# Tuned two-MLP kernel on one Trainium2 core: pairs of token tiles with a lag of three pairs

## What is computed

```python
kv = np.einsum('bhsd,bhse->bhde', k_s, v)          # k_s: softmax over the positions
x  = np.einsum('bhsd,bhde->bhse', q_s, kv)         # q_s: softmax over the columns

h = x @ w_in;  g = np.maximum(h, 0) + alpha * np.minimum(h, 0)
x = g @ w_out

h = x @ w_in2
e = np.exp(h - max(h));  sm = e / (sum(e) + 1e-9)
solu = h * sm
ln = (solu - mean(solu)) / sqrt(var(solu) + 1e-6) * g_ln
out = ln @ w_out2
```

## Time and profile before

| | |
|---|---|
| median of 3 runs | 1238.48 us (1237.42 to 1242.6) |
| profiled execution | 1237.77 us, its span 1236.0 us |
| PE busy in the span | 1196.8 us (97%) |
| DVE, ACT, POOL busy | 909.0 (74%), 537.1 (43%), 310.0 us (25%) |
| ninth chunk's down product | ends at 832.6 us |
| periods of stage 3 | from 832.6 us, the last one begins at 1179.94 us |

### The profile page before, as it was taken

One profiled execution on the slowest core, in us unless ns is written; L12 is line 12 of the kernel. 1 busy time (PEld: TensorE's weight loads), 2 busy tenths in 40 slices (PEclk: granted clock), 3 DMA queues, 4 the chain that ended last, 5 costly groups with the idle time before them and its releaser, 6 DMA issues.

```text
span 1236.0 us, 16164 instructions
## 1 busy us (share of the span) xinstructions
PE 1196.8 (97%) x6013; PEld 988.3 (80%) x6013; DVE 909.0 (74%) x1165; ACT 537.1 (43%) x744; POOL 310.0 (25%) x233
## 2 busy tenths in 40 slices
PE   7999999999999999999999999997889999999997
PEld 6778887878788888888888888985667888888886
DVE  7869678686773577869777686754789888888872
ACT  4443434434353334444434444333454554545441
POOL 5632413224141000000000000124543545353400
PEclk9999999999999999999999999998899999999999
DMA  9797787878865654270642704693355454544333
GB/s 229 226 283 261 238 258 232 249 249 261 268 191 181 236 198 172 74 237 35 196 145 85 238 17 161 207 293 105 125 166 171 150 156 155 152 159 151 135 128 111
DMA packets 211918, 225.07 MB, mean 182 GB/s; under 512 B 63208, under 2 KB 148224, under 8 KB 211712
## 3 DMA queue, kind: packets, MB, share of 16 engines
q1 hardware_dynamic: 206064, 212.50, 54.7%
q0 software_dynamic: 5728, 11.53, 3.3%
q10 hardware_dynamic: 48, 0.01, 0.0%
HBM read 128.51 MB, written 95.48 MB: 181 GB/s over the span
## 4 chain that ended last, share of the span: by engine, by line
PE 77%; DVE 8%; DMA 4%; issue 4%; POOL 2%; SPq 2%; ACT 2%; POOLq 0%; DVEq 0%; ACTq 0%
PE ps_y L1840 8%; PE ps_y L1842 7%; PE ps_y L1841 7%; PE ps_y L1926 5%; PE ps_y L1928 5%; PE ps_y L1930 5%; PE ps_y L1984 5%; PE ps_y L1985 5%; PE ps_y L1986 5%; PE ps_m L1926 3%; PE ps_m L1928 3%; PE ps_m L1930 2%; PE ps_m L1965 2%; PE ps_m L1969 2%; PE ps_m L1967 2%
## 5 line engine op out<-in xcount | busy, mean ns | idle before, releaser
L1840 PE MATMUL ps_y<-X,W 128*128 128x512 f32 x576 | 226.7, 394 | 0.0
L1842 PE MATMUL ps_y<-X,W 128*128 128x512 f32 x576 | 224.4, 390 | 0.0
L1841 PE MATMUL ps_y<-X,W 128*128 128x512 f32 x576 | 224.3, 389 | 0.0
L1364 DVE SCALAR_TENSOR_TENSOR gst<-gst,nslope,ps_y 128x512 f32<-128x512 f32 x144 | 104.4, 732 | 111.0 <-ACT gst L967 110.6
L967 ACT ACTIVATE gst<-ps_y 128x512 f32<-128x512 f32 x144 | 85.7, 596 | 224.8 <-PE ps_y L1842 166.1
L836 POOL TENSOR_TENSOR x2r<-x2r 128x256 f32<-128x256 f32 x18 | 25.1, 1394 | 410.0 <-DMA x2r<-x_scratch 410.0
L1984 PE MATMUL ps_y<-WO,zh 128*128 128x512 f32 x288 | 115.3, 400 | 11.9 <-DVE zl L1665 11.9
L1840 PEld LDWEIGHTS ps_y<-X,W 128*128 128x128 f32 x576 | 108.1, 188 | 23.1
L1842 PEld LDWEIGHTS ps_y<-X,W 128*128 128x128 f32 x576 | 108.1, 188 | 22.8
L1841 PEld LDWEIGHTS ps_y<-X,W 128*128 128x128 f32 x576 | 108.1, 188 | 22.0
L1926 PE MATMUL ps_y<-rh,WOc 128*128 128x512 f32 (+1 forms) x320 | 118.6, 371 | 3.0 <-DVE rl L1526 2.9
(11 more groups left out here) (189 smaller groups left out, 2519.5 us busy)
## 6 DMA issues: line engine op xcount, KB each, us to landing
g_scratch<-gst SPq DMA_DIRECT2D x144, 256.0 KB, 3.5
RX<-g_scratch SPq DMA_DIRECT2D x36, 512.0 KB, 3.6
z_scratch<-zb SPq DMA_DIRECT2D x36, 512.0 KB, 2.7
zt<-z_scratch SPq DMA_DIRECT2D x144, 128.0 KB, 2.9
ws_scratch<-whl SPq DMA_DIRECT2D x22, 512.0 KB, 4.5
RY<-g_scratch SPq DMA_DIRECT2D x18, 512.0 KB, 4.0
RZ<-g_scratch SPq DMA_DIRECT2D x18, 512.0 KB, 4.6
x2r<-x_scratch SPq DMA_DIRECT2D x18, 512.0 KB, 5.0
```

Of the source, the lines that this page charges most:

```text
L1364: nc.vector.scalar_tensor_tensor(gst[:, n % 3, :], gst[:, n % 3, :], nslope[:, f:f + 1], ps_y[:, f % 4, :], ALU.mult, ALU.add).then_inc(g_ ...
L1840: nc.tensor.matmul(o, W1[:, f, 0, a, :], x[:, 0, a, :], start=(a == 0), stop=False)
L1841: nc.tensor.matmul(o, W1[:, f, 0, a, :], x[:, 1, a, :], start=False, stop=False)
L1842: mm = nc.tensor.matmul(o, W1[:, f, 1, a, :], x[:, 0, a, :], start=False, stop=(a == KT - 1))
```

## The change

- TensorE's period n becomes: blocks 0 to 3 of pair n, m2 of (n-3, 0), blocks 4 to 6, m2 of (n-3, 1). Three pairs are behind at the end.
- h has three sets of buffers (hs[n % 3]; h20, h21 are new), so the waits on solu_ok go back three pairs.
- The first five periods of ACT, DVE, POOL and SP stand in another order, and the loops are one pair further behind: DVE's is now zt_low(n-3,0), form_early(n), norm(n-2,0), norm(n-2,1), zt_low(n-3,1), form_12(n), form_21(n), max(n-1,0), max(n-1,1), solu(n-1,0), solu(n-1,1).
- x2r1 and x2lb1 change places in memory. load_x2(1) is issued once the low part of unit (3,1) of the ninth chunk is made; x2_sums(1) stands ahead of load_wo2 on POOL; x2_high(0) comes behind product 2, x2_high(1) behind unit (6,0).
- The ninth chunk's units use three slots. In it DVE does v and c22 behind the low part of unit (4,0), and b_turn of product 4 behind the low parts of product 5.

```diff
-                self.slot = 1 + s % 2 if self.single else r % 3
-                if self.single:
-                    self.before = r - 2 if s >= 2 else r - 3
-                else:
-                    self.before = r - 3
+                self.slot = r % 3
+                self.before = r - 3
...
+                if u == PAIRS:
+                    sp.wait_ge(bl_ok, number(PAIRS, 3, 1) + 1)
+                    load_x2(1)
                 store_x2(u, 3, p1, c22_ok, 2 * (u + 1), y22_st)
...
+            for n in range(5, PERIODS + 4):      # SP
+                if n - 4 < PERIODS:
+                    store_out(n - 4, 1)
+                if n - 2 < PERIODS:
+                    store_z(n - 2, 0)
+                    load_z(n - 2, 0)
+                if n - 3 < PERIODS:
+                    store_out(n - 3, 0)
+                if n - 2 < PERIODS:
+                    store_z(n - 2, 1)
+                    load_z(n - 2, 1)
                 if n + 3 < PERIODS:
                     load_x2(n + 3)
...
             x2_low(0)
+            x2_sums(1)
             load_wo2(0)
             load_wo2(1)
-            x2_sums(1)
             x2_low(1)
             x2_sums(2)
             x2_low(2)
+            x2_sums(3)
             power(0, 0)
-            x2_sums(3)
             x2_low(3)
+            x2_sums(4)
             power(0, 1)
-            x2_sums(4)
+            x2_low(4)
+            x2_sums(5)
             power(1, 0)
-            x2_low(4)
             power(1, 1)
-            x2_sums(5)
+            x2_low(5)
+            x2_sums(6)
             power(2, 0)
             power(2, 1)
-            x2_low(5)
-            x2_sums(6)
-            power(3, 0)
-            power(3, 1)
-            for n in range(5, PERIODS):
-                power(n - 1, 0)
-                power(n - 1, 1)
+            for n in range(5, PERIODS + 2):
+                power(n - 2, 0)
+                power(n - 2, 1)
                 if n + 1 < PERIODS:
                     x2_low(n + 1)
                 if n + 2 < PERIODS:
                     x2_sums(n + 2)
...
+            for n in range(5, PERIODS + 4):      # ACT
+                if n - 2 < PERIODS:
+                    square_tile(n - 2, 1)
+                if n < PERIODS:
+                    first_copy(n)
+                if n - 4 < PERIODS:
+                    out_copy(n - 4, 1)
+                if n - 3 < PERIODS:
+                    zt_high(n - 3, 1)
                 if n + 1 < PERIODS:
                     x2_high(n + 1)
+                if n - 3 < PERIODS:
+                    out_copy(n - 3, 0)
+                if n < PERIODS:
+                    h11_copy(n)
+                if n - 2 < PERIODS:
+                    zt_high(n - 2, 0)
+                if n - 1 < PERIODS:
+                    exp_tile(n - 1, 0)
+                    exp_tile(n - 1, 1)
+                    square_tile(n - 1, 0)
...
+                if t.u == LAST_U and t.k == 4:
+                    if t.j == 0:
+                        post("v", t.u)
+                        post("c22", t.u)
+                    continue
+                if t.u == LAST_U and t.k == 5:
+                    b_turn(UNITS[number(t.u, 4, t.j)])
...
             tile_solu(0, 0)                      # DVE, the first periods
             form_early(1)
-            tile_solu(0, 1)
+            norm_tile(0, 0)
             form_12(1)
             form_21(1)
-            norm_tile(0, 0)
+            form_early(2)
+            tile_solu(0, 1)
+            zt_low(0, 0)
...
+            for n in range(5, PERIODS + 3):
+                zt_low(n - 3, 0)
+                if n < PERIODS:
+                    form_early(n)
+                if n - 2 < PERIODS:
+                    norm_tile(n - 2, 0)
+                    norm_tile(n - 2, 1)
+                zt_low(n - 3, 1)
+                if n < PERIODS:
+                    form_12(n)
+                    form_21(n)
+                if n - 1 < PERIODS:
+                    tile_max(n - 1, 0)
+                    tile_max(n - 1, 1)
+                    tile_solu(n - 1, 0)
+                    tile_solu(n - 1, 1)
...
                 if n >= 3:
-                    m2_product(n - 3, 1)
+                    m2_product(n - 3, 0)
                 for k in range(4, PARTS):
                     m1_product(n, k)
-                if n >= 2:
-                    m2_product(n - 2, 0)
-            m2_product(PERIODS - 3, 1)
-            for n in range(PERIODS - 2, PERIODS):
+                if n >= 3:
+                    m2_product(n - 3, 1)
+            for n in range(PERIODS - 3, PERIODS):
                 for t in range(2):
                     m2_product(n, t)
```

More of the change, by code:

```diff
@@ L112, in linear_attention_two_mlps @@
         h00, h01 = place(RAW_AT + 4096, ("h00", [P, F2], F32), ("h01", [P, F2], F32))
-        zl, p1c, h11t = place(RAW_AT + 6144, ("zl", [P, 2, F2], F32R), ("p1c", [P, TOK], F32), ("h11t", [P, F2], F32))
+        zl, p1c, h11t, h20, h21 = place(RAW_AT + 6144, ("zl", [P, 2, F2], F32R), ("p1c", [P, TOK], F32), ("h11t", [P, F2], F32),
+                                        ("h20", [P, F2], F32), ("h21", [P, F2], F32))
         ps_y = ctx.enter_context(nc.psum_tensor("ps_y", [P, 4, TOK], F32))
@@ L1113, in _ @@
                         c11_copy(t.u)
-                    if t.u == LAST_U and t.k == 4:
+                    if t.u == LAST_U and t.k == 2:
                         x2_high(0)
+                if t.u == LAST_U and t.k == 6 and t.j == 0:
+                    x2_high(1)
             def first_copy(n):
@@ L1168, in _ @@
             exp_tile(0, 0)
+            x2_high(2)
             first_copy(1)
             exp_tile(0, 1)
-            x2_high(2)
             square_tile(0, 0)
             h11_copy(1)
-            square_tile(0, 1)
+            x2_high(3)
             first_copy(2)
-            x2_high(3)
-            exp_tile(1, 0)
             h11_copy(2)
             zt_high(0, 0)
+            square_tile(0, 1)
+            first_copy(3)
+            x2_high(4)
+            exp_tile(1, 0)
             exp_tile(1, 1)
+            zt_high(0, 1)
@@ L1181, in _ @@
             square_tile(1, 0)
-            zt_high(0, 1)
             square_tile(1, 1)
-            first_copy(3)
+            h11_copy(3)
             out_copy(0, 0)
-            x2_high(4)
+            x2_high(5)
             exp_tile(2, 0)
+            first_copy(4)
+            zt_high(1, 0)
             exp_tile(2, 1)
-            zt_high(1, 0)
             out_copy(0, 1)
             square_tile(2, 0)
-            h11_copy(3)
+            zt_high(1, 1)
             square_tile(2, 1)
-            zt_high(1, 1)
+            out_copy(1, 0)
@@ L1195, in _ @@
+            h11_copy(4)
             exp_tile(3, 0)
-            first_copy(4)
-            out_copy(1, 0)
             exp_tile(3, 1)
-            x2_high(5)
+            zt_high(2, 0)
             square_tile(3, 0)
[L1201 to L1213, removed]
+            for n in range(5, PERIODS + 4):
[7 more added lines that the diff above has]
+                    zt_high(n - 3, 1)
@@ L1679, in _ @@
             form_early(1)
-            tile_solu(0, 1)
+            norm_tile(0, 0)
             form_12(1)
             form_21(1)
-            norm_tile(0, 0)
+            form_early(2)
+            tile_solu(0, 1)
+            zt_low(0, 0)
+            form_12(2)
+            form_21(2)
+            norm_tile(0, 1)
+            form_early(3)
             tile_max(1, 0)
-            form_early(2)
-            norm_tile(0, 1)
-            zt_low(0, 0)
             tile_max(1, 1)
             tile_solu(1, 0)
-            form_12(2)
@@ L1691, in _ @@
-            form_21(2)
             tile_solu(1, 1)
+            zt_low(0, 1)
+            norm_tile(1, 0)
+            form_12(3)
+            form_21(3)
+            norm_tile(1, 1)
             tile_max(2, 0)
             tile_max(2, 1)
-            zt_low(0, 1)
-            norm_tile(1, 0)
-            form_early(3)
-            norm_tile(1, 1)
             tile_solu(2, 0)
             zt_low(1, 0)
+            form_early(4)
             tile_solu(2, 1)
-            form_12(3)
-            form_21(3)
@@ L1734, in _ @@
-            n = PERIODS - 1
-            norm_tile(n, 0)
-            norm_tile(n, 1)
-            for t in range(2):
-                zt_low(n - 1, t)
-            for t in range(2):
-                zt_low(n, t)
+            tile_max(3, 0)
+            tile_max(3, 1)
+            tile_solu(3, 0)
+            tile_solu(3, 1)
+            for n in range(5, PERIODS + 3):
[14 more added lines that the diff above has]
+                    tile_solu(n - 1, 1)
```

119 lines of the change are left out of this document (25 added, 94 removed).

## The result

The changed kernel takes **1276.11 us**, the median of 4 runs (1275.45 to 1277.93), beside 1237.95 for the kernel before (1235.40 to 1242.60): ratio 1.031 (95% interval 1.027 to 1.034). It is slower. 1280 in a range of 1240 to 1292 was forecast. The profiled execution took 1275.84 us with a span of 1274.0, 38.0 more than the 1236.0 of before.

What follows compares the result with a forecast made beforehand. TensorE was taken as full through 950 to 1190 us, so only stalls at start and end could be won. 1236.0 - 11.4 (start) + 46.0 (middle) + 7.1 (end) = 1277.7 us of span, stated as 1280, range 1240 to 1292.

Steps and rivals of the forecast that it cites:

- Ninth chunk, +0.7: At unit (4,1), DVE's rl waits for POOL's x2_low(0); TensorE idles 3.6 us in place of 2.9: +0.7 us.
- Start, -25.5 and what is late next: Second pair sooner removes the old start's 25.5 us of stalls; new ones come; start in sum -11.4 us.
- Both new stalls: Start: m2(1,0) waits for zl in period 4, +4.9 and 2.4 clock; m1(2,1) waits for form_12, +4.0 and 1.7.
- Middle, +46.0: Periods 5 to 16: x2_low holds tensor_scalar, zl is late, TensorE idles 2.7 us each, 32.4, plus 13.6 of slow clock.
- the clock's share: Middle: two of three stalls also draw the slow clock, 12 x 1.1 = 13.6 us.
- The bound that only adds 0.41 to tensor_scalar: Middle: tensor_scalar only grows by 0.41, zl is 0.75 us late per period, 9 us in all.
- the second rival: Middle: only the growth of 0.41, zl 0.75 us late per period, total 1242; chance 0.09.
- the first rival: Middle: POOL loses the race, tensor_scalar starts first, zl 1.5 us late, 18 in all, total 1251; chance 0.11.
- x2_low late enough: Middle: rival in which x2_low begins behind zt_low and holds nobody, TensorE never waits, total 1228; chance 0.15.
- End, +7.1: Last products: zl(15,0) and m2(16,0) come late, 11.1 us with slow clock against 4.0 before: +7.1 us.
- m2(16, 0)'s 4.2: End: m2(16,0) waits behind norm(16) twice, maxima and solu of 17: 4.2 us idle.
- The sum, 1279.5: Whole kernel: span 1277.7 us from all terms, 1279.5 for the profiled execution, stated as 1280.

Runs made afterwards that it cites:

- Experiment 6: Changed kernel with load_x2(1), x2_sums(1) and x2_high(1) put back where they stood before the change: 1287.63 us, ratio 1.041.
- experiment 8: experiment 3 plus ACT's exp ahead of zt_high, power(0,0) ahead of x2_sums(3), and x2_low(5) waiting for norm(1,1): 1230.96 us, ratio 0.995.
- experiment 1: Changed kernel, but POOL's x2_low(n+1) waits until DVE's second norm has its e: 1255.65 us, ratio 1.015.
- Experiment 9: experiment 8 with the last period and the end written out in a new order on DVE, ACT and SP: 1220.44 us, ratio 0.987.
- experiment 5: Changed kernel with x2_low as two operations of seven rows each, nothing between them: 1252.49 us, ratio 1.012.
- 10 to 12: x2_low(0), x2_low(1) in four pieces: on Experiment 9 1224.20 us, on the changed kernel 1276.22, on Experiment 9 with waits between pieces 1223.38.
- experiment 11: Changed kernel with x2_low(0) and x2_low(1) in four pieces, nothing between them: 1276.22 us, ratio 1.031.
- experiments 2: Changed kernel with DVE's zt_low(n-3,1) ahead of the two norms: 1255.42 us, ratio 1.014.
- experiment 3: Changed kernel with the edits of experiment 1 and experiments 2 together: 1246.83 us, ratio 1.008.

## Why the prediction was right

By position: unit (4, 0) of the ninth chunk and the first blocks of pairs 5 and 17 begin, in the changed kernel, at

```profile
813.69 0.28 PE L1898 MATMUL ps_m<-rh,WOc 128*128 128x256 f32 x1
...
916.52 0.39 PE L1937 MATMUL ps_m<-W2c,x2hb 128*128 128x512 f32 x1
...
1203.74 0.39 PE L1937 MATMUL ps_m<-W2c,x2hb 128*128 128x512 f32 x1
```

and in the kernel before (pair 17 at 1179.94) at

```profile
810.71 0.28 PE L1926 MATMUL ps_m<-rh,WOc 128*128 128x256 f32 x1
...
935.14 0.39 PE L1965 MATMUL ps_m<-W2c,x2hb 128*128 128x512 f32 x1
```

The kernel before has one product of 5.44 more behind it at that point, so 935.14 stands for 929.70. The start gives 916.52 - 929.70 = -13.2. From pair 5 to pair 17 it is 287.22 in place of 244.80: the middle gives +42.4. Behind that 70.3 in place of 56.1, less the product of 5.44 that moved there: the end gives +8.8. Together 38.0.

- **Ninth chunk, +0.7: right.** POOL first again, this time by 0.31; rl is held 4.80 and TensorE waits 3.4 (forecast 3.6; before 2.9), with 3.41 us at 0.50:

```profile
814.92 4.01 POOL L852 TENSOR_TENSOR x2lb<-x2r,x2hb 128x1792 fp32r<-128x1792 f32 x1
...
815.23 4.80 DVE L1502 TENSOR_TENSOR rl<-RX,rh 128x1024 fp32r<-128x1024 f32 x1
```

- **Start, -25.5 and what is late next.** The wait for p1c is gone. Both new stalls came where they were forecast and for the reasons given: at (2, 1) DVE's norm waited 4.80 for a power that stood behind two POOL jobs, and in period 4 tensor_scalar met x2_low(5):

```profile
857.37 0.57 POOL L857 TENSOR_TENSOR st<-st,mhalf 128x1 f32<-128x1 f32 x1
...
857.97 0.81 DVE L1639 TENSOR_SCALAR e<-e,st 128x1024 f32<-128x1024 f32 x1 [4.80 <-POOL st L857]
...
888.55 4.54 DVE L1639 TENSOR_SCALAR e<-e,st 128x1024 f32<-128x1024 f32 x1 [0.66 <-POOL st L857]
```

  Sizes: 3.3 lost with no slow clock (forecast 4.0 and 1.7), 4.6 and 1.7 (forecast 4.9 and 2.4). The start gained 13.2 in place of 11.4. The changed kernel's profiled execution, though, reached unit (4, 0) 3.0 later. The delay comes from stages that the change doesn't touch: ACT's rounding of the same unit of the down product is 3.3 later at 576.04 already, and in its first 100 us this execution has 10.24 us at clock 0.50 where the one before has 3.41. Over the runs here unit (4, 0) begins at 809.4 to 813.7 us. Without the 3.0 the start gained 16.2, 4.8 more than forecast, 3.4 of it in the sizes above; where the rest comes from isn't shown. Experiment 6 prices the whole edit at 11.5, experiment 8 the two new stalls at 8.5.
- **Middle, +46.0: mechanism right, one term mis-sized.** Twelve stalls, tensor_scalar 4.52 or 4.53 beside x2lb in each. A stall without slow clock costs 2.81 (from 1054.75 to 1077.96 it is 23.21, and a full period is 20.4), against the 2.7 forecast. With slow clock it costs 4.26 (1030.09 to 1054.75). So 12 x 2.81 = 33.7 in place of 32.4. What was off is the clock's share: I took two of three stalls at 1.7, 13.6 us, and it was one of two at 1.45 (in the stretch shown above TensorE ran for 3.11 of the 3.41 us): 6 x 1.45 = 8.7. 33.7 + 8.7 = 42.4, the same as by position. The bound that only adds 0.41 to tensor_scalar is refuted, and with it the second rival; experiment 1 makes the first rival's case and finds its price.
- **x2_low late enough: refuted.** x2lb waits for nothing, as the forecast had it by z's times.
- **End, +7.1: too small by 1.7.** The stalls lose 3.4 (forecast 3.5), 5.3 for m2(16, 0) where 4.2 were forecast, and 1.0 for one that wasn't listed. The clock took 3.1 (forecast 3.4): TensorE ran for 3.41 and 2.86 us at 0.50. Two of the three stalls in the timeline of TensorE, and what stands behind the second on DVE and ACT:

```profile
1227.55 0.56 PE L1956 MATMUL ps_y<-WO,zh 128*128 128x512 f32 x1 [3.24 <-DVE zl L1648]
...
1245.46 0.80 PE L1956 MATMUL ps_y<-WO,zh 128*128 128x512 f32 x1 [5.13 <-DVE zl L1648]
...
1240.63 0.15 DVE L1624 TENSOR_SCALAR st<-st 128x1 f32<-128x1 f32 x1 [4.17 <-ACT e L1125]
...
1238.40 1.06 ACT L1144 ACTIVATE zh<-zt 128x1024 fp32r<-128x1024 f32 x1 [2.88 <-DMA zt<-z_scratch]
```

  The term that was too small is m2(16, 0)'s 4.2. For it the prediction says "the same way" and lists only DVE's work (norms, maxima, solu). In the trace DVE waits 4.17 for ACT's exp(17), which stands behind zt_high(16, 0) and its z from DRAM. Experiment 9, which reorders both engines, takes what the end's stalls lose from 9.7 to 6.5.

The sum, 1279.5, was 3.7 above the profiled execution: middle 3.6 and start 1.8 too high, end 1.7 too low. So a part of the accuracy is luck, errors that cancel; so is the 3.0 of the untouched stages, without which the start would be 4.8 off.

The Trainium skill, page "SBUF — State Buffer", section "Who interferes with whom", gives the exclusive lock for the whole instruction. This case agrees for tensor_scalar, which that section lists among those that can enter a two-port mode (4.53 beside 4.04, 2.60 beside a half), and for the subtraction of two SBUF inputs (4.00 and 4.80). The section also says that VectorE with at most one SBUF input outside these modes doesn't contend; the transpose of 1.25 us beside x2lb in experiment 1 agrees.

## What to carry to other kernels

Where a lag is lengthened to cover one engine's waits, look at what the freed engine now does at once: here POOL's long subtraction no longer waited for its input and so fell on the one DVE instruction in front of TensorE. Such a meeting cost the length of the other engine's operation; order the two by a wait on the idle engine's side, or cut the long operation (which helped in experiment 5 and not in 10 to 12), and then ask which queue stands behind the wait, since here three orders (POOL, DVE, ACT) had to be put right before the middle was full again. Lengthening a lag also moves the end: one more product stands behind the last block, and the order there has to be written for that.

## What the runs showed of the hardware that was not expected

- **Who wins.** With POOL's next operation right behind the one that releases DVE, POOL was first by 0.06 to 0.07 in each of the twelve periods. The held tensor_scalar ended 0.56 behind POOL's operation (1051.68, 1052.24), a held zl of 1024 columns 1.08 behind it (1042.83, 1043.91 in experiment 1).
- **Pieces with nothing between them.** A DVE tensor_tensor was held through four pieces (5.20) and, in experiment 5, through two in the ninth chunk (4.93), while tensor_scalar was let in between two (2.60). With a semaphore wait between pieces tensor_tensor was let in too (2.09). Whether the kind of instruction or something else at that place makes the difference wasn't tried. The price of taking turns: four pieces 7.47 us in place of 4.42.
- **Slow clock.** Of stalls that lose 2.65 us each, at the same spacing, every second one came with 3.41 us at clock 0.50 (seven of the twelve in experiment 11); of those that lose 1.2, 1.3 and 1.7 in the middles of experiments 2, 5 and 1, none; of the two that lose 3.5 and 3.3 in the changed kernel's start, only the first. In experiment 3 one that loses 2.0, at 1027.54, was followed by such a stretch. The length of a stall alone doesn't tell whether the clock falls.
